# Rows of constant matmuls placed between the attention units of the first stage

## The chip, the cores and the metric

The kernel runs on one core of a Trainium2 chip. The metric is the device time of one execution in microseconds (us); lower is better. The core has TensorE (PE, matmuls, with its weight loads listed apart as PEld), VectorE (DVE), ScalarE (ACT), GpSimd (POOL) and SyncE (SP, which issues most DMAs). Each engine runs its own list of instructions in order and waits on semaphores for the others.

## The reference

The reference chains three parts, all in float32. First a linear attention with decay over 4 batches, 8 heads, 768 steps and head size 48:

```python
for t in range(S):
    cur = einsum('bhd,bhe->bhde', u * k[t], v[t])
    y[t] = einsum('bhd,bhde->bhe', r[t], state + cur)
    state = w[t][:, :, :, None] * state + einsum('bhd,bhe->bhde', k[t], v[t])
```

Its output, as 3072 tokens of width 384, is normalised by its root mean square and goes through a gated layer of inner width 1536, `silu(xn @ w_gate) * (xn @ w_val) @ w_out`. The third part is `(s * relu(x @ w_in) ** 2 + b) @ w_out2` with inner width 2048.

## The kernel before, in words

The attention is computed in blocks of 256 tokens (12 blocks, 3 for each batch), two chunks of 128 in each. Inside a chunk the decayed scores are built over seven levels of doubling distance. For every level TensorE multiplies halves of the keys and queries (`level`, line 336, into `level_ps`), DVE places the result in `near` (line 720) and multiplies keys and decays (lines 709 and 702), POOL multiplies the queries (line 864); the next level needs all of these. The last level is `top_level` (line 351). `turn_keys` (line 363) transposes the keys, `attend` (lines 377 and 387) forms the output, `update` (line 400) the new state, and `turn_x` (line 413) transposes the normalised output. These are the attention units. All their operands are plain float32.

The first block of code, `attention_and_gated_phase`, walks over stages `s` from 0 to 6. A stage has 36 places `k`. At each place every engine issues one group of the gated layer for the 512 tokens of the stage before (`gated(s - 1, k)`: gate, value or output matmuls, lines 423 and 435), and then the attention units that belong to that place for the two blocks of this stage (`attention(s, k)`). In stage 0 there is no earlier stage, so TensorE has attention units alone; ACT, DVE and POOL also split the gated layer's weights into a high and a low part there (`w_hi`, `w_lo`). In stages 1 to 5 the gated matmuls stand between the attention units. The gated matmuls' operands are of the type fp32r. `squared_phase` (lines 47 and 1070) then does the third part.

The order of the work is the order of the written code on each engine; there is no planner. `gate_ps` is one bank of PSUM, first used by the first gate group of stage 1. `eye` (128x128) and `u_b` (128x384) are constants that are loaded at the start, together with `g_col`; all three raise `const_in`, on which TensorE waits after `level(0, 0)`.

Of the kernel before, what the change touches and what calls it, by code (L numbers as in the profile page):

```python
# [29 lines left out]
DM = H * D  # L30
# [21 lines left out]
def wait(eng, sem, value):  # L52

    if not isinstance(value, int) or value > 0:
        eng.wait_ge(sem, value)
# [4 lines left out]
STAGED = 5  # L60
WO_PIECES = F1 * DM // PIECE
WIN_PC = KT * FF2 // NBLK
SPLITS = (slice(0, T - P), slice(T - P, T))


# [12 lines left out]
def batch_end(b):  # L78
    return b % BPB == BPB - 1
# [12 lines left out]
def attention_and_gated_phase(nc, a, whole, first, x1_dram, x1_out, x_hi, x_lo, level_ps, mix_ps, gate_ps, value_ps, o_ps):  # L92
# [30 lines left out]
    with ExitStack() as ctx:  # L123
        def sb(name, shape, dt=F32):
            return ctx.enter_context(nc.sbuf_tensor(name, shape, dt, side="right"))
# [13 lines left out]
        u_b = sb("u_b", [P, DM])  # L139
        eye = sb("eye", [P, P])  # L140
# [11 lines left out]
    with ExitStack() as ctx:  # L152
        win_staged = [ctx.enter_context(nc.sbuf_tensor(f"win_staged{i}", [P, WIN_PC], F32, side="right")) for i in range(2)]

# [69 lines left out]
    def _(sp):  # L224
# [33 lines left out]
        def store(g):  # L258
            for j in range(KT):
                wait(sp, x1_done, KT * g + j + 1)  # L260
                sp.dma_start(x1_dram[g][:, j], x1_sb[j % 2][:]).then_inc(x1_out[j % 2], 16)
# [48 lines left out]
        store(NSB - 2)  # L310
        wait(sp, xlo_done, len(SPLITS) * NSB)
        for i in range(2):
# [8 lines left out]
    def _(pe):  # L321
        def level(b, l):
            keys_ready(pe, b, l)
            level_out(pe, b, l - 1)
            for c in range(C):
                if l == 0:
                    pe.wait_ge(r_in[b % 2], (b // 2 + 1) * 16)
                else:
                    wait(pe, rmul_done, C * (LV * b + l - 1) + c + 1)
                for p in range(NP):  # L330
                    q = c * NP + p
                    for i in range(2):
                        for h in range(2):
                            rows = slice(h * SUB, (h + 1) * SUB)
                            cols = slice(q * P + i * SUB, q * P + (i + 1) * SUB)
                            mm = pe.matmul(pairs_ps[i * SUB:(i + 1) * SUB, h * Q + q, 0:HALF], K[b % 2][rows, cols],  # L336
                                           halves(R[b % 2][rows, cols], l)[:, :, 1],
                                           start=True, stop=True, skip_group_check=True)
                mm.then_inc(level_done, 1)

        def top_level(b):

            l = LV - 1
            keys_ready(pe, b, l)
            level_out(pe, b, l - 1)
            wait(pe, rmul_done, C * (LV * b + l - 1) + C)
            for p in range(NP):
                for c in range(C):
                    for h in range(2):
                        rows, q = slice(h * SUB, (h + 1) * SUB), c * NP + p  # L350
                        mm = pe.matmul(pairs_ps[c * SUB:(c + 1) * SUB, h * Q + p], K[b % 2][rows, q * P:q * P + SUB],
                                       R[b % 2][rows, q * P + SUB:(q + 1) * P], start=True, stop=True, skip_group_check=True)
            mm.then_inc(level_done, C)

        def turn_keys(b, c):
            keys_ready(pe, b, LV)
            if c == 0:
                wait(pe, xe_done, KT * C * b)
            else:
                wait(pe, kt_out, turned(b, c))  # L360
            for p in range(NP):
                q = c * NP + p
                mm = pe.transpose(mix_ps[:, p * P:(p + 1) * P], K[b % 2][:, q * P:(q + 1) * P], eye[:])
            mm.then_inc(kt_done, 1)
# [28 lines left out]
        def update(b, c):  # L393
            wait(pe, kt_out, turned(b, c) + 1)
            wait(pe, yo_done, C * b + c + 1)
            pe.wait_ge(v_in, (b + 1) * 16)
            for p in range(NP):
                for h in range(2):
                    head = 2 * p + h
                    mm = pe.matmul(mix_ps[h * SUB:(h + 1) * SUB, p * D:(p + 1) * D],  # L400
                                   KTr[c][:, p * P + h * SUB:p * P + (h + 1) * SUB], v_sb[:, c, head * D:(head + 1) * D],
                                   start=(p == 0), stop=True, skip_group_check=True)
            mm.then_inc(upd_done, 1)
# [12 lines left out]
        def gate_or_value(g, f, j, ps):  # L416
            if f == 0 and j == 0:
                wait(pe, xlo_done, len(SPLITS) * (g + 1))
            if g == 0 and j == 0:
# [7 lines left out]
        def out_tile(g, f):  # L427
            wait(pe, ulo_done, F1 * g + f + 1)
            if g == 0:
                wait(pe, wolo_done, f // 2 + 1)  # L430
            for j in range(KT):
                if f == 0:
                    wait(pe, x1_done, KT * (g - 1) + j + 1)
                for w, x in ((wo_hi, u_hi), (wo_hi, u_lo), (wo_lo, u_hi)):
                    mm = pe.matmul(o_ps[j][:], w[:, f, j * P:(j + 1) * P], x[:, f % 2],  # L435
                                   start=(f == 0 and w is wo_hi and x is u_hi), stop=(f == F1 - 1 and w is wo_lo))
            mm.then_inc(out_done, 1)

        def gated(g, k):
# [7 lines left out]
            else:  # L447
                out_tile(g, f)

        def attention(s, k):  # L450
            b, b2 = 2 * s, 2 * s + 1
            if k in (1, 3, 5, 7, 9):
                level(b, (k + 1) // 2)
            if k == 11:
                top_level(b)
            if k == 13:
                turn_keys(b, 0)
                level(b2, 0)
            if k == 14 and not batch_end(b):
                turn_keys(b, 1)  # L460
            if k == 16:
                attend(b, 0)
            if k == 17:
                update(b, 0)
            if k == 19:
                attend(b, 1)
            if k in (15, 17, 19, 21, 23):
                level(b2, (k - 13) // 2)
            if k == 20 and not batch_end(b):
                update(b, 1)  # L470
            if k == 22:
                turn_x(b, 0)
            if k == 24:
                turn_x(b, 1)
            if k == 25:
                top_level(b2)
            if k == 27:
                turn_keys(b2, 0)
            if k == 28 and not batch_end(b2):
                turn_keys(b2, 1)  # L480
            if k == 29:
                attend(b2, 0)
            if k == 30:
                update(b2, 0)
            if k == 31:
                attend(b2, 1)
            if k == 32 and not batch_end(b2):
                update(b2, 1)
            if k == 33:
                turn_x(b2, 0)  # L490
            if k == 34:
                turn_x(b2, 1)

        for s in range(NSB + 1):
            if s < NSB:
                level(2 * s, 0)
                if s == 0:
                    pe.wait_ge(const_in, CONSTS)
                    pe.wait_ge(pool_zeroed, POOL_ZEROED)
            for k in range(GROUPS):  # L500
                if s > 0:
                    gated(s - 1, k)
                if s < NSB:
                    attention(s, k)
        wait(pe, xlo_done, len(SPLITS) * NSB + 1)
        wait(pe, winlo_done, NBLK)
        wait(pe, silu_done, F1 * NSB)
# [4 lines left out]
    def _(act):  # L512
# [56 lines left out]
        def x_out(b, c):  # L569
            act.wait_ge(const_in, CONSTS)  # L570
            wait(act, xt_done, C * b + c + 1)
            wait(act, xlo_done, len(SPLITS) * (b // 2))
            cols = slice(b % 2 * TB + c * P, b % 2 * TB + (c + 1) * P)
# [4 lines left out]
        def upper_x(s, i):  # L578
            wait(act, xe_done, KT * (2 * C * s + (3, 4)[i]))
            wait(act, value_done, F1 * s)  # L580
            act.activation(x_hi[:, :, SPLITS[i]], x_raw[:, :, SPLITS[i]], ACT.Copy).then_inc(xhi_done, 1)

# [109 lines left out]
    def _(dve):  # L692
# [71 lines left out]
        def lower_x(s, i):  # L764
            wait(dve, xhi_done, len(SPLITS) * s + i + 1)
            dve.tensor_tensor(x_lo[:, :, SPLITS[i]], x_raw[:, :, SPLITS[i]], x_hi[:, :, SPLITS[i]].bitcast(F32),  # L766
                              ALU.subtract).then_inc(xlo_done, 1)
# [86 lines left out]
    def _(pool):  # L854
# [86 lines left out]
        for n in range(NBLK):  # L941
            cols = slice(n * WIN_PC, (n + 1) * WIN_PC)
            pool.wait_ge(win_in[n % 2], (n // 2 + 1) * 16)
# [313 lines left out]
```

## Time and profile before

| | us |
|---|---|
| median of 3 runs | 1125.03 |
| lowest and highest of them | 1123.92, 1126.35 |
| the profiled execution's own time | 1124.27 |
| span of its trace | 1122.5 |
| TensorE busy in the span | 1051.8 (94%) |
| TensorE busy from 0 to 104 us | 57.0 |
| DVE busy in the span | 494.8 (44%) |
| mean granted clock of TensorE | 0.979 |

Stage 0 lasts from the start of the span to about 96 us, where the first gate group begins. A timeline row merges neighbouring instructions of one kind: it gives the start of the first, the time from there to the end of the last, the line, tiles and shape, and how many there are; in brackets stands the idle time of the engine ahead of them and what ended it. The end of a matmul contains its way through the array, so the next one starts before it: the time that a group costs TensorE is read from its start to the start of the next group.

### The profile page before, as it was taken

How to read it: one execution, taken by the hardware profiler on the slowest of the kernel's cores; microseconds unless marked ns; L12 is line 12 of the kernel's file. 1: busy time of each engine (PE TensorE's matmuls, PEld its weight loads, DVE VectorE, ACT ScalarE, POOL GpSimd, SP SyncE). 2: the span in 40 equal slices, each digit the busy share in tenths (PEclk: the TensorE clock that was granted, in tenths of full speed). 3: DMA queues.
4: the chain of work that ended last, by engine and by line, in shares of the span. 5: the costliest groups of instructions: out<-in, count | busy, mean ns of one | idle time of the engine just before them, and what ended most of it. 6: DMA issues, size and time to landing. Idle time of an engine off the chain costs nothing. (4 is left out here: it accounts for less than half of the span.)

```text
span 1122.5 us, 24796 instructions
## 1 busy us (share of the span) xinstructions
PE 1051.8 (94%) x10512; PEld 887.3 (79%) x10512; DVE 494.8 (44%) x686; ACT 384.7 (34%) x701; POOL 289.7 (26%) x291
## 2 busy tenths in 40 slices
PE   3657999899999999998999899999999999999998
PEld 3556777678777877786788688689899898989988
DVE  5745562545265426543654222292532506143250
ACT  1443324332423342343234321362432505143240
POOL 6743542443145214430543062040000000000000
PEclk9957999999999999999999999999999999999999
DMA  7422231111112111211200040130101010010000
GB/s 266 138 95 67 73 113 40 62 66 65 53 49 67 62 53 49 67 63 52 64 15 16 11 141 20 56 113 22 36 15 42 0 45 11 21 35 7 21 0 28
DMA packets 21982, 62.26 MB, mean 55 GB/s; under 512 B 2817, under 2 KB 6273, under 8 KB 21889
## 3 DMA queue, kind: packets, MB, share of 16 engines
q1 hardware_dynamic: 21600, 60.31, 15.9%
q8 instruction: 72, 1.18, 0.4%
q10 hardware_dynamic: 288, 0.61, 0.1%
q14 instruction: 22, 0.17, 0.1%
HBM read 51.46 MB, written 9.44 MB: 54 GB/s over the span
## 5 line engine op out<-in xcount | busy, mean ns | idle before, releaser
L864 POOL TENSOR_TENSOR R<-R,WB 128x256 f32<-128x256 f32 x168 | 149.8, 911 | 244.4 <-issue 77.8
L1151 DVE SCALAR_TENSOR_TENSOR sqr<-relu,sb_col 128x512 f32<-128x512 f32 x96 | 80.8, 843 | 209.3 <-ACT relu L1102 207.8
L336 PEld LDWEIGHTS level_ps<-R,K 64*64 64x64 f32 x4608 | 83.0, 148 | 43.9 <-issue 23.6
L780 DVE TENSOR_TENSOR u<-value_ps,silu 128x512 f32<-128x512 f32 x72 | 49.8, 691 | 145.4 <-PE value_ps L423 145.4
L336 PE MATMUL level_ps<-R,K 64*64 64x32 f32 x4608 | 91.0, 232 | 24.3 <-DVE near L720 13.4
L709 DVE TENSOR_TENSOR K<-K,WB 128x512 f32<-128x512 f32 x84 | 70.9, 844 | 88.7 <-PE level_ps L336 65.1
L600 ACT ACTIVATE silu<-gate_ps 128x512 f32<-128x512 f32 x72 | 43.0, 597 | 187.5 <-PE gate_ps L423 187.4
L435 PE MATMUL o_ps<-u_hi,wo_hi 128*128 128x512 f32 x216 | 90.6, 419 | 12.7 <-DVE u_lo L784 12.6
L606 ACT ACTIVATE u_hi<-u 128x512 fp32r<-128x512 f32 x72 | 45.5, 632 | 159.9 <-DVE u L780 159.9
L1070 PE MATMUL o_ps<-wt_hi,g_lo 128*128 128x384 f32 x288 | 96.2, 334 | 0.0
L1070 PE MATMUL o_ps<-wt_hi,g_hi 128*128 128x384 f32 x288 | 96.2, 334 | 0.0
L1070 PE MATMUL o_ps<-wt_lo,g_hi 128*128 128x384 f32 x288 | 96.2, 334 | 0.0
L423 PE MATMUL gate_ps<-x_hi,w_hi 128*128 128x512 f32 x216 | 91.0, 421 | 0.9 <-DVE x_lo L766 0.9
L423 PE MATMUL value_ps<-x_hi,w_hi 128*128 128x512 f32 x216 | 88.7, 410 | 0.0
L435 PE MATMUL o_ps<-u_lo,wo_hi 128*128 128x512 f32 x216 | 86.3, 400 | 0.0
L423 PE MATMUL gate_ps<-x_lo,w_hi 128*128 128x512 f32 x216 | 86.3, 399 | 0.0
L423 PE MATMUL gate_ps<-x_hi,w_lo 128*128 128x512 f32 x216 | 86.1, 399 | 0.0
L435 PE MATMUL o_ps<-u_hi,wo_lo 128*128 128x512 f32 x216 | 85.9, 398 | 0.0
L423 PE MATMUL value_ps<-x_lo,w_hi 128*128 128x512 f32 x216 | 85.5, 396 | 0.0
L423 PE MATMUL value_ps<-x_hi,w_lo 128*128 128x512 f32 x216 | 85.4, 395 | 0.0
L784 DVE TENSOR_TENSOR u_lo<-u,u_hi 128x512 fp32r<-128x512 f32 x72 | 73.6, 1022 | 23.2 <-ACT u_hi L606 23.2
L1156 DVE SCALAR_TENSOR_TENSOR g_lo<-sqr,sb_col,g_hi 128x512 fp32r<-128x512 f32 x96 | 73.7, 768 | 1.7 <-ACT g_hi L1093 0.9
(104 smaller groups left out, 2001.6 us busy)
## 6 DMA issues: line engine op xcount, KB each, us to landing
kr_nat<-kr SPq DMA_DIRECT2D x12, 768.0 KB, 4.1
K<-kT SPq DMA_DIRECT2D x12, 512.0 KB, 3.5
WB<-wT SPq DMA_DIRECT2D x12, 512.0 KB, 4.1
R<-rT SPq DMA_DIRECT2D x11, 512.0 KB, 3.5
v_sb<-v SPq DMA_DIRECT2D x12, 384.0 KB, 3.5
staged<-wgv SPq DMA_DIRECT2D x12, 384.0 KB, 4.4
x_scratch<-x_sb SPq DMA_DIRECT2D x18, 256.0 KB, 2.2
x_raw<-x_scratch SPq DMA_DIRECT2D x6, 768.0 KB, 4.4
```

The costliest lines, as they stand in the source:

```text
L336: mm = pe.matmul(pairs_ps[i * SUB:(i + 1) * SUB, h * Q + q, 0:HALF], K[b % 2][rows, cols], halves(R[b % 2][rows, cols], l)[:, :, 1], start ...
L423: mm = pe.matmul(ps[:], w[:, f, j, k], x[:, k], start=(k == 0 and w is w_hi and x is x_hi), stop=(k == KT - 1 and w is w_lo))
L435: mm = pe.matmul(o_ps[j][:], w[:, f, j * P:(j + 1) * P], x[:, f % 2], start=(f == 0 and w is wo_hi and x is u_hi), stop=(f == F1 - 1 and w ...
L600: act.activation(silu[f % 2][:], gate_ps[:], ACT.Silu).then_inc(silu_done, 1)
L606: act.activation(u_hi[:, f % 2], u[f % 2][:], ACT.Copy).then_inc(uhi_done, 1)
L709: dve.tensor_tensor(k, k, decay(l, 1), ALU.mult).then_inc(kmul_done, 1)
L780: dve.tensor_tensor(u[f % 2][:], value_ps[:], silu[f % 2][:], ALU.mult).then_inc(u_done, 1)
L784: dve.tensor_tensor(u_lo[:, f % 2], u[f % 2][:], u_hi[:, f % 2].bitcast(F32), ALU.subtract).then_inc(ulo_done, 1)
L864: pool.tensor_tensor(q, q, decay(l, 0)[:, c * per_c:(c + 1) * per_c], ALU.mult).then_inc(rmul_done, 1)
L1070: mm = pe.matmul(o_ps[t][:, 0:DM], g[:, f, t * P:(t + 1) * P], w[:, f], start=(f == 0 and g is g_hi and w is wt_hi), stop=(f == F2 - 1 and ...
L1151: dve.scalar_tensor_tensor(out=sq[f % 2][:], in0=relu[f % 2][:], scalar=sb_col[:, 0:1], in1=relu[f % 2][:], op0=ALU.mult, op1=ALU.mult).th ...
L1156: dve.scalar_tensor_tensor(out=g_lo[:, f], in0=sq[f % 2][:], scalar=sb_col[:, 1:2], in1=g_hi[:, f].bitcast(F32), op0=ALU.add, op1=ALU.subt ...
```

## The change

A function `keep_busy(n)` issues n matmuls of the constant `u_b` against the constant `eye`, 128 rows, 128 columns of weights and 384 moving columns each, into the bank `gate_ps`, whose content nobody reads before the first gate group overwrites it. Eight of them follow `level(0, 0)` and the wait on `const_in`; a table `BUSY` says how many follow each place `k` of stage 0. It is 8 + 107 = 115 matmuls. Nothing else is changed, and no other engine's list.

```diff
+BUSY = {1: 6, 3: 6, 5: 6, 7: 6, 9: 6, 11: 3, 13: 2, 14: 7, 15: 2, 16: 4, 17: 2, 19: 2, 20: 6, 21: 2, 22: 2, 23: 2,
+        24: 2, 25: 4, 27: 4, 28: 4, 29: 3, 30: 4, 31: 3, 32: 9, 33: 4, 34: 6}
...
+        def keep_busy(n):
+
+            for _ in range(n):
+                pe.matmul(gate_ps[:, 0:DM], eye[:], u_b[:], start=True, stop=True, skip_group_check=True)
...
                 if s == 0:
                     pe.wait_ge(const_in, CONSTS)
                     pe.wait_ge(pool_zeroed, POOL_ZEROED)
+                    keep_busy(8)
             for k in range(GROUPS):
                 if s > 0:
                     gated(s - 1, k)
                 if s < NSB:
                     attention(s, k)
+                if s == 0:
+                    keep_busy(BUSY.get(k, 0))
```

TensorE's list at the start of the program, before. The names are line, operation, output tile, its operands, shape of the moving operand, and how many matmuls as the program writes them:

```order
L320 UNCONDITIONAL_BRANCH
L336 MATMUL level_ps<-R,K 64x32 x192
L351 MATMUL level_ps<-R,K 64x64 x16
L363 MATMUL mix_ps<-eye,K 128x128 x4
L336 MATMUL level_ps<-R,K 64x32 x32
```

And the same place in the changed kernel, where these functions stand two lines further down (`level` is line 338) and the matmul of `keep_busy` is line 455:

```order
L338 MATMUL level_ps<-R,K 64x32 x32
L455 MATMUL gate_ps<-u_b,eye 128x384 x8
L338 MATMUL level_ps<-R,K 64x32 x32
L455 MATMUL gate_ps<-u_b,eye 128x384 x6
L338 MATMUL level_ps<-R,K 64x32 x32
L455 MATMUL gate_ps<-u_b,eye 128x384 x6
```

The six levels of the first block stood in one row; now eight constant matmuls stand behind the first, and six behind each of the others.

TensorE's list at the end of stage 0, from the last `attend` to the first gate group, before:

```order
L387 MATMUL mix_ps<-v_sb,scores 64x48 x16
L400 MATMUL mix_ps<-v_sb,KTr 64x48 x8
L413 MATMUL mix_ps<-eye,y 128x128 x6
L336 MATMUL level_ps<-R,K 64x32 x32
L423 MATMUL gate_ps<-x_hi,w_hi 128x512
```

And in the changed kernel:

```order
L389 MATMUL mix_ps<-v_sb,scores 64x48 x16
L455 MATMUL gate_ps<-u_b,eye 128x384 x3
L402 MATMUL mix_ps<-v_sb,KTr 64x48 x8
L455 MATMUL gate_ps<-u_b,eye 128x384 x9
L415 MATMUL mix_ps<-eye,y 128x128 x3
L455 MATMUL gate_ps<-u_b,eye 128x384 x4
L415 MATMUL mix_ps<-eye,y 128x128 x3
L455 MATMUL gate_ps<-u_b,eye 128x384 x6
L338 MATMUL level_ps<-R,K 64x32 x32
L425 MATMUL gate_ps<-x_hi,w_hi 128x512
```

Each unit at the end of the stage has a row of 3 to 9 constant matmuls behind it, and the first gate group stands behind all of them.

## Rows read from the trace of the kernel before

**Rows 1.** The page's second part: TensorE's granted clock in 40 slices of the span, in tenths.

```profile
PEclk9957999999999999999999999999999999999999
```

**Rows 2.** Busy time, instructions and granted clock by stretch of stage 0.

```profile
core 0: us, PE busy (x) PEld busy (x) DVE busy (x) ACT busy (x) POOL busy (x), PEclk, DMA share, GB/s
12.70:55.90 43.20, 24.64 (x648) 22.77 (x648) 31.16 (x32) 15.29 (x24) 35.95 (x29) 1.00 0.51 180
55.90:59.40 3.50, 2.14 (x105) 1.91 (x104) 2.83 (x5) 0.00 (x0) 1.71 (x3) 1.00 0.76 245
59.40:86.70 27.30, 16.30 (x290) 14.04 (x283) 10.86 (x18) 12.81 (x27) 10.68 (x12) 0.50 0.19 69
86.70:90.20 3.50, 0.46 (x13) 0.33 (x10) 0.51 (x2) 1.34 (x4) 0.89 (x2) 0.99 0.81 242
90.20:96.20 6.00, 3.68 (x71) 2.85 (x71) 3.15 (x5) 3.38 (x8) 1.58 (x2) 0.50 0.02 8
```

**Rows 3.** Timeline of TensorE through stage 0 and into stage 1.

```profile
12.74 1.93 PE L336 MATMUL level_ps<-R,K 64*64 64x32 f32 x64 [4.19 <-DMA g_col<-g]
...
26.08 1.93 PE L336 MATMUL level_ps<-R,K 64*64 64x32 f32 x64 [2.83 <-DVE near L720]
...
49.95 1.09 PE L400 MATMUL mix_ps<-v_sb,KTr 128*64 128x48 f32 x16 [2.52 <-issue]
...
56.00 1.14 PE L336 MATMUL level_ps<-R,K 64*64 64x32 f32 x64
57.07 0.67 PE L400 MATMUL mix_ps<-v_sb,KTr 128*64 128x48 f32 x16
...
90.53 0.91 PE L413 MATMUL mix_ps<-eye,y 128*128 128x128 f32 x3 [3.37 <-DVE y L762]
...
96.17 0.79 PE L423 MATMUL gate_ps<-x_hi,w_hi 128*128 128x512 f32 x1 [0.86 <-DVE x_lo L766]
...
100.17 0.52 PE L423 MATMUL value_ps<-x_hi,w_hi 128*128 128x512 f32 x1
...
102.49 1.14 PE L336 MATMUL level_ps<-R,K 64*64 64x32 f32 x64
```

**Rows 4.** The same group of line 377, cut at 53.056, 53.10 and 53.22 us.

```profile
52.84 0.58 PE L377 MATMUL mix_ps<-state_bd,R 128*64 128x96 f32 x3
...
52.84 0.59 PE L377 MATMUL mix_ps<-state_bd,R 128*64 128x96 f32 x4
...
52.84 0.75 PE L377 MATMUL mix_ps<-state_bd,R 128*64 128x96 f32 x6
```

**Rows 5.** The transposes of line 363 at 37 us, cut after two and three.

```profile
37.03 0.69 PE L363 MATMUL mix_ps<-eye,K 128*128 128x128 f32 x2 [0.90 <-DVE K L709]
...
37.03 0.90 PE L363 MATMUL mix_ps<-eye,K 128*128 128x128 f32 x3 [0.90 <-DVE K L709]
```

**Rows 6.** Timeline of TensorE in the third part, where the operands are fp32r.

```profile
849.81 0.33 PE L1070 MATMUL o_ps<-wt_hi,g_hi 128*128 128x384 f32 x1
849.98 0.33 PE L1070 MATMUL o_ps<-wt_lo,g_hi 128*128 128x384 f32 x1
```

**Rows 7.** Timeline of TensorE in stage 1: the attention units at the full clock.

```profile
134.67 0.60 PE L363 MATMUL mix_ps<-eye,K 128*128 128x128 f32 x4
135.20 1.14 PE L336 MATMUL level_ps<-R,K 64*64 64x32 f32 x64
...
148.04 0.67 PE L400 MATMUL mix_ps<-v_sb,KTr 128*64 128x48 f32 x16
148.64 1.14 PE L336 MATMUL level_ps<-R,K 64*64 64x32 f32 x64
...
154.08 0.88 PE L377 MATMUL mix_ps<-state_bd,R 128*64 128x96 f32 x16
154.79 1.09 PE L387 MATMUL mix_ps<-v_sb,scores 128*64 128x48 f32 x32
155.81 1.14 PE L336 MATMUL level_ps<-R,K 64*64 64x32 f32 x64
```

## The prediction, written before the changed kernel ran

> **What bounds the kernel now.** I read the page's slices first. TensorE is the engine that ends the span, and the granted clock leaves the full rate only in the first tenth of it [rows 1]: the third and the fourth slice of 28 us stand at 0.5 and 0.7. So whatever the change can give lies in stage 0, up to the first gate group at 96.17 us [rows 3]. The view of stretches then shows the stage in numbers [rows 2]: from 12.70 to 96.20 us TensorE is busy 24.64 + 2.14 + 16.30 + 0.46 + 3.68 = 47.2 us and idle 36.3 us. The timeline shows what the idle is: waits of 2 to 3.4 us for the placing of the last level by DVE, for the normalised y and the like, between units of 1 to 2 us [rows 3]. The stage is a chain that goes back and forth between TensorE and the others; no engine is full in it.
>
> The clock column needs care. The stretch from 12.70 to 55.90 us says 1.00 [rows 2], but the 64 instructions of one level take 1.93 us at 12.74 and at 26.08 us and 1.14 us at 56.00 us [rows 3]. So the array ran at its lower level (1.2 GHz) from the start, and the 1.00 there stands only because no record came before the first rise near 56 us. It rose near 56 us after TensorE had worked without a gap from 49.95 us, fell near 59.5 us, was full again only from 86.8 to 90.2 us, in which TensorE did almost nothing, and for good from 100.4 us. In effect nearly all of stage 0's 47 us of TensorE work is done at 1.2 GHz.
>
> **What the change adds.** 115 matmuls, each 128 rows by 128 weight columns by 384 moving columns, plain float32, all in TensorE's list; no wait, no DMA, nothing on other engines. They are cheap only where TensorE would have waited anyway, because the list is in order: a unit that is ready stands behind the row of constants in front of it. So the price of one decides.
>
> The price of one. The program's row of a level has 32 matmuls and the trace has 64 instructions [rows 3], so a plain float32 matmul is two instructions: 230 are added. For what one instruction costs there are rows on two sides:
> - From below: fp32r instructions with the same 384 moving columns follow each other after 0.17 us (849.81 to 849.98) [rows 6]. If a plain instruction passes its columns once too, a matmul costs 2 x 0.173 = 0.35 us at the full clock.
> - From above: in the group of line 377, with 96 moving columns at 1.2 GHz, the third and the fourth instruction are both there between 53.05 and 53.10 us and their ends are 0.01 us apart; two more bring the end from 0.59 to 0.75 us [rows 4]. The two work side by side in two halves of the array's columns, and the pair takes 0.16 us = 192 cycles of 1.2 GHz, twice its 96 columns. A transpose of 128 plain columns, which has the whole array, adds 0.90 - 0.69 = 0.21 us = 256 cycles [rows 5], again two for each column. So a plain instruction passes its columns twice: 768 cycles, 0.32 us at the full clock and 0.64 us at the lower one, and a matmul of two instructions 0.64 us or 1.28 us.
>
> I take the upper one, since both plain rows say so and the lower one is a row of another type; with the small addition that stands between pairs of line 377 (0.71 us for 8 pairs at the full clock [rows 7], 0.089 where 0.080 is the bare stream) I use 0.65 us.
>
> The Trainium skill says in FP8 and Floating Point Precision, section TensorE Precision Notes, that true FP32 takes four passes through the array, high and low parts of both operands. By that rule a constant matmul is 4 x 384 / 2.4 GHz = 0.64 us, and the reading from below is excluded; the rows of lines 377 and 363 agree with it (0.16 us a pair, 0.21 us a transpose), while no row of before has a plain float32 matmul with the whole array.
>
> **Do they fit into the waits?** Place by place, at 0.65 us: six of them are 3.9 us behind each level of the first block, where the waits were at most 2.83 us [rows 3]; nine are 5.9 us in front of `turn_x`, where the wait was 3.37 us [rows 3]; four are 2.6 us in front of `update` of the first chunk, where it was 2.52 us [rows 3]. Behind the levels at places 15 to 23 TensorE mostly had no wait at all, and two stand there each time. The eight at the start come when `const_in` rises, at the moment at which level 1 started at once (12.74 us, the wait ended by g_col [rows 3]), so nothing covers them. Every row is at least as long as the wait it lies in. So TensorE never waits again in stage 0 and becomes the bound of it, and its end is a plain sum of TensorE's work:
>
> - start at 12.7 us (`const_in`, unchanged);
> - 115 x 0.65 = 74.8 us of constants;
> - the real units at the full clock, since TensorE is without gaps. By starts: a level 1.07 us (56.00 to 57.07) [rows 3], and there are 12 of them up to and with `level(2, 0)` = 12.8; the two top levels 0.7 each (half the instructions of a level, and a tail) = 1.4; four `turn_keys` and four `turn_x` at 0.53 = 4.2; three of line 377 at 0.71 = 2.1; four of line 387 at 1.02 = 4.1; four of line 400 at 0.60 = 2.4 [rows 7]. Sum 27.0 us;
> - the clock is at its lower level when the dense work begins. It rose 6.1 us after the dense stretch that began at 49.95 us [rows 3]; 6 us at half rate lose 3 us.
>
> 12.7 + 74.8 + 27.0 + 3.0 = 117.5 us for the first gate group, against 96.17: 21.3 us later.
>
> **What comes back.** The first gate and value group ran mostly at the lower clock: 96.17 to 102.49 us, 6.3 us for 18 matmuls. The last nine of them took 102.49 - 100.17 = 2.3 us with the first still slow [rows 3], so all 18 at the full clock take at most 4.6 us, and I take 4.3. It gives back 2.0 us. The wait of 0.86 us for x_lo in front of it [rows 3] is inside the sum already. Behind stage 0 nothing changes: the weights' splits on ACT, DVE and POOL get more time, but TensorE did not wait for them. The profiled execution's 1124.3 + 21.3 - 2.0 = 1143.6 us; it lies 0.8 us under the median of the runs, so I say 1143.5 us, 1.7% slower.
>
> Its own range: at the bare 0.64 us the constants are 73.6 us and the rise may come after 4 us, which gives 1141; with the 0.0133 us that fp32r instructions take above their 0.160 us of stream, added to each of two passes [rows 6], a matmul is 0.69 us and the sum 5 us more, and some us of switching between groups on top: 1151. On the other side some waits can be shorter than thought where DVE and POOL get in each other's way less: 1138.
>
> **Rivals.**
> 1. The constants pass once per instruction, 0.35 us each, and the change pays. Then rows of six (2.1 us) lie inside the level waits, and the units on the chain go from 47.2 us at the lower clock to 27.0 us, 20.2 us gained. Against it: 8 uncovered at the start, at the lower clock, 8 x 0.69 = 5.5 us; the six pairs at places 13, 15, 17, 19, 22 and 23 where TensorE had no wait, 6 x 0.7 = 4.2 us; about 3.5 us where three to seven stand in a shorter wait; 1 us until the clock is up. Net 6, and 2 from the first gate group: 8 us faster, 1116 us. It decides from the point where one costs less than about 0.45 us: (1143.6 - 1116) over 0.65 - 0.35 is 92 us for each us of price, so 1124 is met at 0.44 us. For it speaks that the rows of six, seven and nine would nearly fill the waits of 2 to 3.4 us; against it stand the plain rows [rows 4, 5]. Chance 9%. The Trainium skill says in TensorE: Matmul & The Clock Gate, section Why this matters for your kernels, that TensorE should be kept busy without long idle gaps between bursts, since it falls back to the half clock in them; by that rule alone the change is right and this rival's time comes out. The rows agree with the rule (1.93 us in the gapped stretches, 1.14 us after a dense one), but it says nothing of a filler's own price.
> 2. The constants don't lift the clock, and everything stays at 1.2 GHz: 115 x 1.28 = 147 us and 47.2 us of units from 12.7 us on, the gate group at 207 us, 1235 us in all. Against it: plain float32 units without a gap did raise it at 56 us [rows 3]. Chance 2%.
> 3. A part of the stage stays at the lower level, because a wait of some us is left somewhere, and the clock falls once or twice for some us: each us at half clock costs half a us, so 3 to 10 us on the forecast, 1147 to 1154. Chance 10%.
> 4. The rows lie beside waits and the clock gains just what they cost: the time stays, 1123 to 1127. It needs a price near 0.44 us, for which no row speaks. Chance 2%.
>
> **Chances.** The forecast has 77%, rival 1 9%, rival 2 2%, rival 3 10%, rival 4 2%. Under 0.2% (2 us) nothing can be told from no change. Slower: 77 + 2 + 10 = 89%; same 2%; faster 9%. The range that leaves out the faster rival and the ends of the others is 1136 to 1152 us.
>
> **What the profile after would show.** Line 455 with 230 instructions, 0.32 us from start to start; a row of six from one level to the next as 3.9 us and a level's period of 5 us instead of 3.9 to 4.9; levels at 1.14 us from about 19 us on; granted clock 1.00 recorded from about 19 to 104 us; no idle of TensorE worth naming between 12.7 us and the first gate group, which starts near 117 us; other engines waiting for TensorE where it had waited for them. The forecast is wrong if line 455's instructions follow each other after 0.16 to 0.17 us, or if TensorE still waits for DVE between the rows of constants.

## The result and the profile after

The changed kernel takes 1150.55 us (median of 4 runs, 1148.68 to 1152.05) against 1124.64 us of the kernel before (4 runs): the ratio is 1.0232, 95% interval 1.0218 to 1.0245. It is slower, by 26 us. The prediction was 1143.5 us, between 1136 and 1152, with 89% for slower. The profiled execution took 1152.05 us, the longest of the four, with a span of 1150.3 us.

The page's slices and stretches answer to [rows 1, 2] (the columns are those of rows 2):

```profile
PE   6999999899989998999899989999999999999999
PEclk9999999999999999999999999999999999999999
```

```profile
12.40:80.70 68.30, 65.97 (x934) 41.86 (x935) 39.12 (x45) 17.82 (x31) 41.50 (x36) 1.00 0.43 148
80.70:87.60 6.90, 6.90 (x75) 4.29 (x74) 2.15 (x3) 2.63 (x6) 1.24 (x2) 0.51 0.00 0
87.60:124.08 36.48, 36.48 (x324) 23.04 (x323) 6.32 (x12) 12.43 (x28) 6.25 (x8) 1.00 0.13 41
```

TensorE, idle for 36 of 84 us before, is idle for 2.3 us between 12.4 and 124.1 us. The clock column shows one stretch of 6.9 us at the lower level. Its 1.00 at the start of the stage is again no full clock: the first 16 constant instructions took 7.08 us (12.41 to 19.49), where 16 at the full clock are 5.2 us. What TensorE waits for in that time is down to two waits; the first two rows are the start of the program, as before:

```profile
PE level_ps L338 <- DMA R<-rT: 6.3, 1, 6.3
PE gate_ps L455 <- DMA g_col<-g: 4.2, 1, 4.2
PE mix_ps L415 <- DVE y L772: 1.9, 1, 1.9
PE mix_ps L365 <- DVE K L719: 0.4, 1, 0.4
```

The timeline of TensorE, against [rows 3]:

```profile
12.41 7.15 PE L455 MATMUL gate_ps<-u_b,eye 128*128 128x384 f32 x16 [4.20 <-DMA g_col<-g]
19.49 1.14 PE L338 MATMUL level_ps<-R,K 64*64 64x32 f32 x64
20.55 4.14 PE L455 MATMUL gate_ps<-u_b,eye 128*128 128x384 f32 x12
24.62 1.14 PE L338 MATMUL level_ps<-R,K 64*64 64x32 f32 x64
...
70.32 0.67 PE L402 MATMUL mix_ps<-v_sb,KTr 128*64 128x48 f32 x16
70.92 4.14 PE L455 MATMUL gate_ps<-u_b,eye 128*128 128x384 f32 x12
74.99 1.14 PE L338 MATMUL level_ps<-R,K 64*64 64x32 f32 x64
76.06 1.56 PE L455 MATMUL gate_ps<-u_b,eye 128*128 128x384 f32 x4
79.52 0.62 PE L415 MATMUL mix_ps<-eye,y 128*128 128x128 f32 x3 [1.91 <-DVE y L772]
...
81.88 1.94 PE L338 MATMUL level_ps<-R,K 64*64 64x32 f32 x64
...
109.88 6.07 PE L455 MATMUL gate_ps<-u_b,eye 128*128 128x384 f32 x18
115.79 0.50 PE L415 MATMUL mix_ps<-eye,y 128*128 128x128 f32 x3
...
124.08 0.50 PE L425 MATMUL gate_ps<-x_hi,w_hi 128*128 128x512 f32 x1
...
128.47 1.14 PE L338 MATMUL level_ps<-R,K 64*64 64x32 f32 x64
```

The reader is to see four things. A level takes 1.14 us from 19.49 us on, so the clock is up. From one level to the next it is 5.13 us (19.49 to 24.62), where it was 3.9 to 4.9 us. The first gate group starts at 124.08 us, 27.9 us later than at 96.17 us [rows 3]. And it gives 1.9 us back: to the next level it is 4.39 us instead of 6.32 us. That leaves 26.0 us at the level of 128.47 us; the other 1.8 us of the span's 27.8 us come later. There this execution has the clock at 0.50 in four stretches of 3.4 us (from 231.0, 340.2, 558.6 and 753.2 us), the one before in three (from 312.1, 639.7 and 725.1 us); the last section has more on them.

### The profile page after: what moved, and what is told of

It is laid out like the page before. It is cut to its first block and busy times, and to the rows that moved or that the text cites. A ratio compares the mean times of both kernels' runs of the same rounds, so it can differ in the third digit from the quotient of the medians.

```text
span 1150.3 us, 25256 instructions
## 1 busy us (share of the span) xinstructions
PE 1113.9 (97%) x10742; PEld 914.1 (79%) x10742; DVE 492.9 (43%) x686; ACT 384.8 (33%) x701; POOL 289.5 (25%) x291
## 5 line engine op out<-in xcount | busy, mean ns | idle before, releaser
L437 PE MATMUL o_ps<-u_hi,wo_hi 128*128 128x512 f32 x216 | 91.3, 423 | 12.6 <-DVE u_lo L794 12.6
L338 PEld LDWEIGHTS level_ps<-R,K 64*64 64x64 f32 x4608 | 75.6, 137 | 29.9 <-issue 23.0
L338 PE MATMUL level_ps<-R,K 64*64 64x32 f32 x4608 | 83.6, 223 | 6.3 <-DMA R<-rT 6.3
L455 PE MATMUL gate_ps<-u_b,eye 128*128 128x384 f32 x230 | 84.5, 514 | 4.2 <-DMA g_col<-g 4.2
```

The costliest lines, as they stand in the source:

```text
L455: pe.matmul(gate_ps[:, 0:DM], eye[:], u_b[:], start=True, stop=True, skip_group_check=True)
```

## The experiments

Each compares with the kernel before, which ran beside it on the same chip: 1123.81 us for the first four, 1123.97 us for the next four, 1124.17 us for the last two. Two variants of different sets, and a variant with the changed kernel, are best compared by their ratios; 0.001 is 1.1 us.

**Half width.** Every constant moves 192 columns instead of 384.

```diff
-                pe.matmul(gate_ps[:, 0:DM], eye[:], u_b[:], start=True, stop=True, skip_group_check=True)
+                pe.matmul(gate_ps[:, 0:DM // 2], eye[:], u_b[:, 0:DM // 2], start=True, stop=True, skip_group_check=True)
```

> The constants move 192 columns instead of 384, same places and counts. Theory (a row costs what it takes beyond the wait it lies in, and the clock that it holds up pays): one instruction about 0.18 us from start to start, a constant matmul 0.36 us, 115 of them 41 us; most rows then lie in waits, levels take 1.14 us, and the first gate group starts near 89 us instead of 124 us; faster than before, 1114 to 1120 us. Rival (a raised clock is worth nothing on this chain, because it goes back and forth between engines, and rows only cost): half of the loss of the full width is left, 1130 to 1138 us.

Measured: 1124.12 us against 1123.81 us, ratio 1.0002 (0.9991 to 1.0014): no difference. Both expectations missed. The timeline shows the first gate group at 98.71 us, where 89 us were expected, and where the gain stayed away:

```profile
12.34 5.32 PE L455 MATMUL gate_ps<-u_b,eye 128*128 128x192 f32 x16 [4.00 <-DMA g_col<-g]
17.58 1.14 PE L338 MATMUL level_ps<-R,K 64*64 64x32 f32 x64
...
25.17 1.16 PE L338 MATMUL level_ps<-R,K 64*64 64x32 f32 x64 [0.85 <-DVE near L730]
...
29.94 1.14 PE L338 MATMUL level_ps<-R,K 64*64 64x32 f32 x64 [1.47 <-DVE near L730]
...
38.28 0.69 PE L353 MATMUL level_ps<-R,K 64*64 64x64 f32 x32 [1.63 <-POOL R L874]
```

The eight at the start cost 5.2 us (12.34 to 17.58). From level 1 to the top level it is 20.7 us, against 22.3 us before (12.74 to 34.99): the five levels are 0.8 us shorter each, which would be 4 us, but DVE and POOL, not TensorE, set the pace there, and the full clock brought 1.6 us. Then the clock fell: it is 0.50 from 58.4 to 65.0 us, and the row of six at 61.23 us takes 4.12 us where the others take 2.22 us. From the level of place 21 to the gate group it is 33.4 us (65.28 to 98.71) instead of 37.1 us. So what the second half gained paid for the start, for the fall of the clock and for the rows that lie in no wait. (The profiled execution took 1126.44 us, 2.3 us above the median.)

**Quarter width.** The same with 96 columns.

> The constants move 96 columns. Theory: a constant matmul 0.20 us, 23 us in all, all rows inside waits or nearly; if the clock still rises early and stays, the first gate group starts near 86 us and the time is 1108 to 1114 us; if the thinner rows don't hold the clock up, levels take 1.93 us in stretches and the time is 1115 to 1122 us. Rival (a raised clock is worth nothing): 1124 to 1130 us.

Measured: 1127.55 us, ratio 1.0033 (1.002 to 1.0046): slower than before by 0.3%. The theory failed on price and on clock:

```profile
15.90 1.93 PE L338 MATMUL level_ps<-R,K 64*64 64x32 f32 x64
17.77 2.87 PE L455 MATMUL gate_ps<-u_b,eye 128*128 128x96 f32 x12
20.57 1.93 PE L338 MATMUL level_ps<-R,K 64*64 64x32 f32 x64
...
42.74 1.93 PE L338 MATMUL level_ps<-R,K 64*64 64x32 f32 x64
```

The levels stay at 1.93 us up to the one at 42.74 us, although TensorE has no wait from 12.2 to 48 us, and a row of six costs 2.80 us, 0.47 us for each constant instead of the 0.20 us expected. So an unbroken list alone did not lift the clock. The rival's range held the time, but for another reason: for most of the first half the clock was not raised.

**No row at the start.** The call `keep_busy(8)` is left out, all else at full width.

> The eight constants behind the first level are left out, all others stay at full width. Theory (nothing covers the eight, 12.41 to 19.49 us): level 1 starts at 12.4 us instead of 19.5 us, and all of stage 0 is 6 to 7 us earlier, 1143.5 to 1145 us; the clock rises in the rows behind level 1 instead. Rival (the eight are what lifts the clock, so that without them the levels stay at 1.93 us and rows at twice their time): 1155 us or more.

Measured: 1145.02 us, ratio 1.0194 (1.018 to 1.0209), less than the changed kernel by 5.5 us (medians) or 4.3 us (ratios) where 6 to 7 were expected. Level 1 starts at 12.33 us, its row of six still takes 5.6 us because the clock is not up yet, and from level 2 (19.80 us, instead of 24.62) on it is like the changed kernel up to the first `turn_x`. The theory holds in kind: the eight were uncovered. It is a little too large in size, since without them level 1 and its row run at the lower clock, so that 4.8 of the 7.1 us are left at level 2.

**The longest row doubled.** 18 instead of 9 at place 32.

```diff
-        24: 2, 25: 4, 27: 4, 28: 4, 29: 3, 30: 4, 31: 3, 32: 9, 33: 4, 34: 6}
+        24: 2, 25: 4, 27: 4, 28: 4, 29: 3, 30: 4, 31: 3, 32: 18, 33: 4, 34: 6}
```

> 18 instead of 9 constants at place 32, in front of turn_x. Theory (TensorE is the bound there, each further constant matmul costs its full 0.678 us): 6.1 us more than the changed kernel, 1156.5 us. Rival (some of the row still lies beside the wait for the normalised y): less than 4 us more, under 1154.5 us.

Measured: 1154.56 us, ratio 1.028 (1.0265 to 1.0294): more than the changed kernel by 4.0 us (medians) or 5.4 us (ratios) where 6.1 was expected and the rival had less than 4. By these neither reading is clear. The row itself is:

```profile
107.64 11.88 PE L455 MATMUL gate_ps<-u_b,eye 128*128 128x384 f32 x36
119.36 0.50 PE L415 MATMUL mix_ps<-eye,y 128*128 128x128 f32 x3
```

From its start to `turn_x` it is 11.72 us against 5.91 us (109.88 to 115.79): 5.81 us for 18 more instructions, 0.323 us each, all of it uncovered. So the price in the row was right, 0.645 us for a constant. The rest came from elsewhere: in this profile the clock did not fall near 80 us, though the wait of 1.91 us ahead of `turn_x` is there too. From `turn_x` to the last `update` it took 26.55 us (80.49 to 107.04) and in the changed kernel's profile 29.76 us (79.52 to 109.28), 3.2 us more, with the lower clock from 80.7 to 87.6 us.

**Half width without the row at the start.**

> Half-width constants (192 columns), without the eight behind the first level. Theory (the half-width kernel paid 5.2 us for those eight, from 12.34 to 17.58 us, and part of that is lost again because its first row then runs at the lower clock): 2 to 4 us faster than half width with them, 1120 to 1122 us. Rival (without the eight the clock rises late and the levels fall back to 1.93 us): no gain or a loss against half width, 1124 us or more.

Measured: 1120.24 us, ratio 0.9977 (0.9961 to 0.9993), less than half width with the eight by 3.9 us (medians) or 2.8 us (ratios), and just faster than before. As the theory had it.

**Late rows, cut to the waits.** Half width, none at the start, and rows only in the second half of the stage, each shorter than the wait that the kernel before had at its place.

```diff
+BUSY = {20: 3, 21: 7, 25: 4, 27: 5, 28: 1, 29: 1, 30: 3, 31: 1, 32: 9, 33: 2, 34: 2}
...
-                    keep_busy(8)
```

> Half-width constants from place 20 on alone, 38 of them, in rows cut to be shorter than the wait that the kernel before shows at the place. Theory (in the second half of the stage the other engines are mostly idle and TensorE's units are the chain, so the full clock there pays once no row is longer than its wait): from the level at 59 us to the first gate group 28 to 30 us instead of 37 us, then 2 us less for that group, 1112 to 1116 us. Rival (a raised clock is worth nothing on the chain): 1123 to 1126 us.

Measured: 1118.57 us, ratio 0.9965 (0.9951 to 0.9978): faster than before by 0.35%, and 2.6 us above the expected range. Its timeline:

```profile
59.09 1.13 PE L337 MATMUL level_ps<-R,K 64*64 64x32 f32 x64 [0.19 <-issue]
60.15 2.54 PE L454 MATMUL gate_ps<-u_b,eye 128*128 128x192 f32 x14
63.92 0.62 PE L414 MATMUL mix_ps<-eye,y 128*128 128x128 f32 x3 [1.22 <-DVE y L770]
...
68.07 0.69 PE L352 MATMUL level_ps<-R,K 64*64 64x64 f32 x32 [1.83 <-POOL R L872]
...
82.72 3.19 PE L454 MATMUL gate_ps<-u_b,eye 128*128 128x192 f32 x18
86.16 0.62 PE L414 MATMUL mix_ps<-eye,y 128*128 128x128 f32 x3 [0.25 <-DVE y L770]
...
91.52 0.51 PE L424 MATMUL gate_ps<-x_hi,w_hi 128*128 128x512 f32 x1 [1.31 <-DVE x_lo L774]
```

From the level at 59.09 us to the gate group it is 32.4 us instead of 37.1 us; 28 to 30 were expected. Part of the gain turned into longer waits: the top level now waits 1.83 us for POOL (0.53 us for DVE before), and the gate group 1.31 us for x_lo (0.86 us before), since TensorE arrives earlier than they do. The row behind the top level runs at the lower clock, which is 0.50 from 69.6 to 73.0 us.

**Rows cut to the waits in both halves.** The same, and rows of five at places 1 to 9, 14 and 16, one at 11.

> The same, with half-width rows of five in the first half of the stage as well (places 1 to 9, 14 and 16, one at 11), none behind the first level. Theory (there DVE and POOL are the chain, so the full clock gives little): 0 to 2 us faster than the late rows alone, 1111 to 1115 us. Rival (the full clock is worth the same per level everywhere, 0.8 us for each of the dozen units there): 6 us or more faster than the late rows alone, under 1108 us.

Measured: 1118.3 us, ratio 0.9956 (0.9942 to 0.997), the lowest of all, but above the 1111 to 1115 us expected and only 0.3 us from the late rows alone, inside either's interval. The first half gave 4.1 us by the profiles (the level of place 21 at 55.02 instead of 59.09 us, and the gate group at 87.39 instead of 91.52 us), more than the 2 us expected; 2.6 us of it are given back later (the spans are 1114.4 and 1115.9 us), mostly at the ends of stages 1 and 2, where this execution's clock fell and the other's did not.

**One row moved.** Full width, 115 constants, but the six of place 20 stand behind the level of place 21.

```diff
-BUSY = {1: 6, 3: 6, 5: 6, 7: 6, 9: 6, 11: 3, 13: 2, 14: 7, 15: 2, 16: 4, 17: 2, 19: 2, 20: 6, 21: 2, 22: 2, 23: 2,
+BUSY = {1: 6, 3: 6, 5: 6, 7: 6, 9: 6, 11: 3, 13: 2, 14: 7, 15: 2, 16: 4, 17: 2, 19: 2, 21: 8, 22: 2, 23: 2,
```

> The changed kernel at full width with its 115 constants, but the six of place 20 moved behind the level of place 21 (eight stand there then). Theory (the 1.91 us for which TensorE waits ahead of turn_x, and the lower clock from 80.8 us, are there because the row stands in front of the level on which the normalised y hangs): the wait is gone and mostly the fall of the clock as well, 2 to 5 us faster than the changed kernel, 1145.5 to 1148.5 us. Rival (TensorE is full, so the place of a row is indifferent): 1150 to 1151 us.

Measured: 1146.48 us, ratio 1.0207 (1.0187 to 1.0228), less than the changed kernel with the same work by 4.1 us (medians) or 2.8 us (ratios). The two intervals overlap at their ends, so the size is not sharp. The profile is:

```profile
70.97 1.14 PE L338 MATMUL level_ps<-R,K 64*64 64x32 f32 x64
72.04 5.43 PE L455 MATMUL gate_ps<-u_b,eye 128*128 128x384 f32 x16
77.31 0.50 PE L415 MATMUL mix_ps<-eye,y 128*128 128x128 f32 x3
```

The wait for y is gone, `turn_x` starts at 77.31 us instead of 79.52 us, and the level behind it takes 1.14 us, not 1.94 us. So the wait of the changed kernel came from the place of the six: DVE normalises y behind the work on the level of place 21, and the row of place 20 held that level back. The changed kernel's DVE list shows it standing idle for the level:

```profile
76.29 0.71 DVE L719 TENSOR_TENSOR K<-K,WB 128x512 f32<-128x512 f32 x1 [3.82 <-PE level_ps L338]
76.92 0.71 DVE L730 COPY_PREDICATED near<-masks,level_ps 128x512 f32<-128x512 uint8 x1
77.53 2.26 DVE L772 TENSOR_SCALAR y<-y,rinv 128x384 f32<-128x384 f32 x2
```

With the row moved y is begun at 74.92 us instead of 77.53 us, and the clock does not fall in the rest of the stage.

**Late rows at full width.** 15 full-width constants in rows about as long as the late half-width ones.

```diff
+BUSY = {20: 1, 21: 3, 25: 2, 27: 2, 30: 1, 32: 4, 33: 1, 34: 1}
```

> The late rows alone, but with full-width constants (384 columns), 15 of them, so that each row is about as long as with 38 half-width ones. Theory (what counts is the length of a row against its wait, not the width of a constant): the same as the late half-width rows, first gate group at 90 to 92.5 us, 1117 to 1120.5 us. Rival (a full-width constant does harm of its own): 1123 us or more.

Measured: 1120.67 us (12 runs), ratio 0.9969 (0.9956 to 0.9983), with the gate group at 90.84 us. The ratio is that of the late half-width rows. Between these two widths, what matters is how long a row is against its wait, not how wide a constant is.

**Early rows alone.** Half width, only at places 1 to 16.

> Half-width rows in the first half of the stage alone (places 1 to 16), none later. Theory (there the full clock moves the chain by about 4 us up to the level at 59 us, as the kernel with rows in both halves showed, and the second half then runs at the lower clock as in the kernel before): level of place 21 near 55 us instead of 59.1 us, first gate group 92 to 93 us, 1120 to 1122 us. Rival (the gain of the first half is eaten by later waits, DMAs or the splits of the weights): 1123 to 1125 us.

Measured: 1121.84 us (12 runs), ratio 0.9979 (0.9966 to 0.9992), inside the expected range. The level of place 21 starts at 56.68 us (55 was expected) and the gate group at 93.96 us (92 to 93). The rows did not hold the clock up all the time there:

```profile
26.07 1.14 PE L337 MATMUL level_ps<-R,K 64*64 64x32 f32 x64 [1.74 <-DVE near L728]
27.13 3.54 PE L454 MATMUL gate_ps<-u_b,eye 128*128 128x192 f32 x10
30.60 1.14 PE L337 MATMUL level_ps<-R,K 64*64 64x32 f32 x64
31.67 1.89 PE L454 MATMUL gate_ps<-u_b,eye 128*128 128x192 f32 x10
```

The same row of five takes 3.54 us at the lower clock and 1.89 us at the full one; a wait of 1.74 us stood ahead of the slow one.

## Why the prediction was right, and what it mis-sized

**What bounds the kernel: right.** The clock column's 1.00 before 56 us was no full clock; levels went from 1.93 to 1.14 us once it was truly raised. That TensorE becomes the bound of stage 0 is shown by the 109.35 us of busy time in 111.7 us, and by the doubled row, of whose addition nothing was covered.

**The price of a constant: right.** Two instructions of 0.323 us, so the reading with two passes of the columns for each instruction holds (768 cycles are 0.320 us) and rival 1's price of 0.35 us a constant is out for this kernel.

**The sum: 117.5 us was forecast for the gate group, 124.08 us came.** By terms, from the timeline:

| | forecast | measured | difference |
|---|---|---|---|
| start | 12.7 | 12.4 | -0.3 |
| constants | 74.8 | 230 x 0.3225 = 74.2, and 4.1 above it in 27 rows | +3.5 |
| lower clock at the start | 3.0 | 7.08 - (16 x 0.323 + 0.20) = 1.7 | -1.3 |
| waits left | 0 | 1.91 + 0.41 = 2.3 | +2.3 |
| fall of the clock at 80.7 us | 0 | 3.2, against the profile of the doubled row | +3.2 |
| the units at the full clock | 27.0 | 26.2 | -0.8 |

The sum of the last column is 6.6 us. The loss at the start differs between executions: for the same 16 instructions it was 1.7 us here and 2.8 us in the profile of the doubled row (12.33 to 20.46 us). The term that no row of before had is what a row of constants takes above its instructions: 20.55 to 24.62 us is 4.07 us, and 12 x 0.3225 is 3.87, so 0.20 us ahead of a level; 109.88 to 115.79 us is 5.91 us against 18 x 0.3225 = 5.81, so 0.10 us ahead of transposes. Over 27 rows that is about 4 us, of which the forecast's 0.65 us a constant held only 0.6 us.

**"TensorE never waits again": wrong, in one place that mattered.** The step said that every row is at least as long as the wait it lies in, and that TensorE mostly had no wait behind the levels at places 15 to 23. The kernel before has one there, between the level of place 21 and `turn_x`:

```profile
63.94 0.91 PE L413 MATMUL mix_ps<-eye,y 128*128 128x128 f32 x3 [3.18 <-DVE y L762]
```

The row of place 21 is two constants, 1.3 us against 3.18 us, and 1.91 us of wait were left. The six of place 20 stand ahead of the level and can't cover it; they delay its cause. By the forecast's own sign of being wrong, TensorE still waiting for DVE between the rows, this step failed. With the six moved behind the level, both the wait and the fall of the clock are gone and the gate group starts at 118.55 us, 5.5 us earlier in the profiles and 1.1 us from the forecast's 117.5. In the runs it is 2.8 to 4.1 us. That the wait alone makes the clock fall is not shown: the doubled row's profile has the same wait and no fall there, and the profile without the eight has the same wait and a fall of half the length (0.50 from 75.5 to 78.7 us).

**The time came by rival 3's way.** A wait left somewhere and a clock that falls for some us were the forecast's third rival, with 1147 to 1154 us and a chance of 10%, and that is what the changed kernel's profile shows. Its 1150.55 us lie inside the stated range because the range reached into this rival's, 7 us above the point that was forecast. The slowdown was 26 us and not 19. The direction and the mechanism were right; that the number fell inside the range is in part luck. A slip went with it: the profiled execution lay 0.8 us under the median, so the sum's 1143.6 us meant 1144.4 us for the median, not 1143.5.

**What comes back, 2.0 us: right** (1.9 us). **"Behind stage 0 nothing changes": nearly.** Up to 168 us every level lies 25.98 or 25.99 us later. From 206 us on it is 27.2 to 27.7 us, from 533 us on 29.2 us, and the spans differ by 27.8 us; the two larger steps lie where the clock fell in the changed kernel's execution alone (231.0 and 558.6 us).

**Rival 1's mechanism was half there.** Half width is close to its test: a constant costs 0.325 us there (four more instructions ahead of a transpose take 0.65 us more, at 76.91 against 70.25 us), in the same places. The rival had 8 us faster for 0.35 us; the ratio came as 1.0002. So the time of no change is met near 0.33 us and not at 0.44. The rival counted the units' whole 20.2 us as gained; a good part of it was the other engines' time (1.6 us of 4 in the first block), and its clock fell again, from 58.4 to 65.0 us. With the half-width rows in all places and none at the start the gain is 3.7 us by the medians and 2.6 us by the ratio; with rows cut to the waits it is 5.7 and 4.9 us. The intervals of these two overlap, so that cutting the rows pays by itself is likely and not shown.

## What to carry to other kernels

A filler (an instruction whose result nobody needs) in an in-order list costs its whole time beyond the wait that it lies in. So price it from its operand type first: here a float32 matmul is two instructions with two passes each. Then cut each row below its wait. Put it behind the instruction that the waited-for engine needs, not in front: a row ahead of the cause moves the wait along. Where the other engines set the pace, part of what a faster TensorE clock gives turns into new waits: in the first half of the stage here the profiles show 2.4 to 4.1 us, in the second 4.6 us. And compare the prize with the price: the full-width rows cost 26 us, the best ones gained 5 to 6 us of 1124.

## What the runs showed of the hardware that was not expected

- In the quarter-width profile TensorE has no wait from 12.2 to 48 us, and the array stayed at the lower clock, with levels at 1.93 us up to 42.74 us. With 192 and 384 columns in the same places the level at 17.58 and at 19.49 us already took 1.14 us. Each instruction of a quarter-width row took 0.23 us (2.80 us for 12) where 2 x 96 columns are 0.16 us at 1.2 GHz. Weight loads are busy for 18.06 of the 19.00 us from 16 to 35 us there; that they set this floor is likely but was not tried.
- Each end of the stages 1 to 5 has a wait of 2.5 us for `u_lo` (five waits, 12.6 us in all, before and after). In some executions the clock falls behind it and in others not, with the same code there. From the execution with rows in both halves, in stage 1, the granted clock and then the wait ahead of it:

```profile
193.90:197.20 3.30, 3.30 (x9) 2.27 (x7) 0.63 (x2) 0.00 (x0) 0.00 (x0) 0.50 0.00 0
```

```profile
193.51 0.56 PE L436 MATMUL o_ps<-u_hi,wo_hi 128*128 128x512 f32 x1 [2.51 <-DVE u_lo L792]
```

  The execution with late rows alone has the same wait, 2.52 us at 197.64 us, and the full clock behind it:

```profile
198.00:201.40 3.40, 3.40 (x75) 2.72 (x74) 0.86 (x3) 1.08 (x2) 0.67 (x1) 1.00 0.02 5
```

  The first of the two executions lost 1.6 us against the other from the last level ahead of this place to the next behind it. It is of the size of the spread between runs of one kernel (2 to 4 us), and differences of 1 to 2 us between the last variants are not told apart from it.
